# Attention with block turns: both scores of a slot ahead of the sums, sums in four visits, the norm a slot later, bias rows of the next heads first in the queue

## Chip, cores and metric

The kernel runs on one core of a Trainium2 chip. The metric is the device time of one launch in microseconds (us).

## What is computed

Attention with a position bias over 4 batches, 8 heads, 576 positions and a head size of 64, then two expert layers. Only the attention is touched here:

```
scores = q @ k.T / sqrt(D) + bias[head]        # 576 x 576 for each of 32 (batch, head)
attn   = exp(scores - max) / sum
out    = attn @ v
```

The bias depends on the head and on the two positions, not on the batch. A first stage of the kernel computes it for all heads and writes it to DRAM (`bias_ihj`).

## The kernel before, in words

**Pairs and passes.** Two heads of one batch form a pair; there are 16 pairs, and four pairs in a row (the four batches) share the bias rows of their two heads. Every engine runs `pair(p, ...)` for p = 0 to 15; the text calls one such call *pass p*. Passes 0, 1, 14 and 15 are written out, passes 2 to 13 are a loop of two passes a turn. Engines meet only through semaphores.

**Slots.** The 576 query rows of the two heads are cut into nine units of 128 rows: slots 0 to 3 hold one unit for each head, slot 4 (`MIX`) holds the last 64 rows of both. Work is one slot ahead: pass p makes slots 1, 2, 3 and MIX of pair p, then slot 0 of pair p+1. Under the same pass the weighted sums with V of pair p-1 are made.

**The steps of a unit**, with the lines of the profile:

- TensorE `scores` (L438): four matmuls for a unit, eight for MIX, into one of two PSUM buffers (h = 0, 1). A unit can start when the unit that used its buffer last has been read by VectorE.
- VectorE `add_bias` (L589): adds the bias, takes the row maximum, writes `a_sc` and `a_nmax`. The text calls it an *add*.
- ScalarE `exps` (L647): the exponential with its row sums, into `a_pr`.
- VectorE `turn` (L601): transposes 32 x 32 blocks of `a_pr` into `a_pt`.
- TensorE `values` (L547): the sums with V over 18 blocks of keys, 16 rows of the trace each. `VISITS` says in which slots of the pass which blocks are done. The first visit waits for V, for the turns of its pair, and for the norm of the pair before (`s_x`), whose PSUM banks it writes.
- ScalarE `keep_out` (L655, L661) copies the finished sums to `a_ot`, TensorE `turn_back` (L559) turns them into banks 4 and 5, and VectorE `normal` (L617, two products, the *norm*) multiplies them by the inverse row sums (L610, L611) into `a_xp`, which SyncE stores to `x_tokens`.

**GpSimd** splits q and k of a later pair in two parts (`split_k`, `split_q`, L367 to L387).

**SyncE's queue** issues all transfers in the order of the code: in pass p the q and k of pair p+2, in passes 3, 7 and 11 the five bias tiles of the next two heads (`load_bias`, L334, L331), the stores of pair p-1, and V of pair p+1 (`load_v`, L324). Each transfer of q, k or V is 288 KB, four for q and k of a pair and four for its V.

Of the kernel before, what the change touches and what calls it, by code (L numbers as in the profile page):

```python
# [275 lines left out]
def front_stages(sem, arena, psum, qt, kt, vt, ww, wg, biasd, xd, ident, rt, small):  # L276
# [7 lines left out]
    VISITS = {1: range(0, 6), 2: range(6, 12), 3: range(12, NK)}  # L284
# [161 lines left out]
    def sync(e):  # L446
# [18 lines left out]
        def pair(p, u, uses):  # L465
            if isinstance(p, int) and p == 0:
                load_v(e, 0, 0)
                load_v(e, 1, 1)
            if not (isinstance(p, int) and p >= NPAIR - 2):
                split_done(e, p)  # L470
                load_qk(e, p + 2, u)
            if not isinstance(p, int) and u == 1:
                with e.If(uses % 2 == 1):
                    for s in range(SLOTS):
                        e.wait_ge(s_b, sem.at(s_b, p * TPP + min(2 * s + 2, TPP)))
                        sem.apart(e, p)
                        load_bias(e, (p // B + 1) % (H // 2), s)
            if from_pair(p, 1):
                store_first(p - 1, 1 - u)
                if not (isinstance(p, int) and p == NPAIR - 1):  # L480
                    e.wait_ge(s_o, sem.at(s_o, p))
                    sem.apart(e, p)
                    load_v(e, p + 1, 1 - u)
                store_second(p - 1, 1 - u)

        each_pair(e, pair)
        store_first(NPAIR - 1, 1)
        store_second(NPAIR - 1, 1)
# [40 lines left out]
    def tensor(e):  # L529
# [34 lines left out]
        def pair(p, u, uses):  # L564
            for s in range(SLOTS):
# [3 lines left out]
                if s in VISITS and from_pair(p, 1):  # L569
                    values(p - 1, 1 - u, uses - 1 + u, VISITS[s])  # L570
                if exists(np_) and ns != MIX:
                    scores(e, np_, nu, nuses, ns, 1)
                if s == MIX and from_pair(p, 1):
                    turn_back(p - 1)
# [6 lines left out]
    def vector(e):  # L581
# [21 lines left out]

        def normal(p, u, uses, half):
# [3 lines left out]
            if half == 0:  # L608
                e.wait_ge(s_e, sem.at(s_e, p * TPP + TPP))
                e.reciprocal(rinv[:, u, 0:TPP], sums[:, u, :]).then_inc(s_r, 1)  # L610
                e.reciprocal(rinv[:, u, TPP:TPP + 1], sums[:, u, TPP - 1:TPP]).then_inc(s_r, 1)  # L611
# [9 lines left out]
        def pair(p, u, uses):  # L621
            for s in range(SLOTS):
# [3 lines left out]
                if exists(np_) and ns != MIX:  # L626
                    add_bias(np_, nu, nuses, ns, 1)
                turn(p, u, s)
                if s == MIX and from_pair(p, 1):
# [1186 lines left out]
```

## Time and profile before

| | |
|---|---|
| median of 3 runs | 1091.58 us (1091.49 to 1092.24) |
| profiled execution: its time, its span | 1093.94 us, 1092.1 us |
| busy over the span: TensorE, VectorE, ScalarE, GpSimd | 1006.4, 790.5, 413.6, 202.6 us |
| attention, from the first scores to the last norm | about 61 to 357 us of the span |
| mean granted TensorE clock | 0.966 |

Times in the rows are microseconds from the start of the span. PE is the matmul side of TensorE, PEld its weight loads, DVE is VectorE, ACT ScalarE, POOL GpSimd, and SPq SyncE's queue. The ends of matmuls are modelled by the profiler, their starts are not.

A row of busy time by stretch has the stretch, its length, then busy time and count of instructions of PE, PEld, DVE, ACT and POOL, the granted TensorE clock (1.00 is full), the busy share of the DMA engines, and GB/s.

A pass is counted here from the start of the add of its slot 1, head 0, to the same add of the next pass. These adds start at 77.51 us (pass 1), 123.89 (3), 230.77 (9), 246.11 (10), 313.54 (14) and 330.11 (15). The `turn_back` of pass 15 starts at 343.84 us.

### The profile page before, as it was taken

What the parts mean: (1) busy time and instruction counts of PE and PEld (TensorE: products, weight loads), DVE (VectorE), ACT (ScalarE), POOL (GpSimd) and SP (SyncE); (2) the same over time, 40 slices, a digit from 0 to 9 for tenths busy, and PEclk for the clock granted to TensorE, in tenths of its full rate; (3) what the DMA queues carried; (4) which work ended last, traced back from release to release, by engine and by line L of the source; (5) the groups of instructions that cost most, each with busy time, mean ns of one, the idle gap of its engine ahead of it and who ended that gap; (6) DMA issues with size and microseconds to landing.
All of it is one profiled execution on the core that took longest, in us unless ns stands there. A gap on an engine that the chain in (4) does not pass through costs nothing.

```text
span 1092.1 us, 28659 instructions
## 1 busy us (share of the span) xinstructions
PE 1006.4 (92%) x10409; PEld 913.6 (84%) x10410; DVE 790.5 (72%) x1268; ACT 413.6 (38%) x783; POOL 202.6 (19%) x195
## 2 busy tenths in 40 slices
PE   5876779798787999999999999999999999999997
PEld 2355667677677899999999999999999999999996
DVE  8985668688685845765656489878776777777765
ACT  7873445455453334644444244231121212112111
POOL 2025234525450231221212000001010100100101
PEclk9987989899898989999999999999999999999999
DMA  4886678878763581561512170002000100100000
GB/s 146 284 238 130 139 209 191 219 171 182 211 148 68 195 281 52 204 204 50 204 50 89 63 258 1 1 1 80 29 29 0 50 8 0 58 0 0 29 1 29
DMA packets 68078, 117.43 MB, mean 108 GB/s; under 512 B 28384, under 2 KB 39696, under 8 KB 65984
## 3 DMA queue, kind: packets, MB, share of 16 engines
q1 hardware_dynamic: 64000, 103.45, 33.9%
q0 software_dynamic: 4032, 13.37, 3.6%
q8 instruction: 28, 0.46, 0.2%
q14 instruction: 18, 0.15, 0.0%
HBM read 91.41 MB, written 25.40 MB: 107 GB/s over the span
## 4 chain that ended last, share of the span: by engine, by line
PE 65%; DVE 2%; issue 1%; ACT 1%; POOL 1%; DMA 0%; POOLq 0%; DVEq 0%; ACTq 0%
PE psum L1688 27%; PE psum L1696 13%; PE psum L1201 11%; PE psum L1210 10%; PE psum L1187 1%; PE psum L547 1%; DVE f_eg L1643 0%; PE psum L1249 0%; DMA e_xin<-x_tokens,e_col 0%; PE psum L559 0%; PE psum L831 0%; PE psum L849 0%; PE psum L438 0%; POOL e_xin L1153 0%; POOL e_col L1149 0%
## 5 line engine op out<-in xcount | busy, mean ns | idle before, releaser
L1643 DVE RECIPROCAL f_eg<-f_eg 128x384 f32<-128x384 f32 x72 | 183.3, 2545 | 0.0
L647 ACT ACTIVATE a_pr<-a_sc,a_nmax 128x576 f32<-128x576 f32 x144 | 111.3, 773 | 142.0 <-DVE a_nmax L589 96.1
L1611 ACT ACTIVATE f_eg<-psum 128x384 f32<-128x384 f32 x72 | 35.4, 492 | 312.0 <-PE psum L1688 312.0
L589 DVE CUSTOM_DVE_ANT_0 a_sc<-psum,a_bias 128x576 f32<-128x576 f32 x144 | 104.8, 743 | 65.3 <-PE psum L438 47.6
L1688 PE MATMUL psum<-f_x,f_ghi 128*128 (+1 forms) x576 | 147.5, 337 | 0.4 <-DVE f_x L1504 0.4
L1688 PE MATMUL psum<-f_x,f_vhi 128*128 (+1 forms) x576 | 146.1, 334 | 0.0
L438 PE MATMUL psum<-a_khi,a_qs 128*128 128x288 f32 x320 | 104.4, 345 | 34.7 <-DVE a_nmax L589 30.4
L438 PEld LDWEIGHTS psum<-a_khi,a_qs 128*128 128x128 f32 x320 | 65.1, 204 | 56.8 <-DVE a_nmax L589 40.8
L1688 PEld LDWEIGHTS psum<-f_x,f_ghi 128*128 128x128 f32 x576 | 105.8, 188 | 6.6 <-DVE f_x L1504 0.6
L547 PE MATMUL psum<-a_pt,a_v 32*64 32x128 f32 (+1 forms) x4608 | 102.0, 312 | 9.6 <-issue 8.8
L1580 POOL DMA_INDIRECT out<-f_ob,f_cols x18 | 18.1, 1007 | 464.9 <-ACT f_ob L1597 316.3
L547 PEld LDWEIGHTS psum<-a_pt,a_v 32*64 32x64 f32 x4608 | 86.3, 140 | 21.2 <-issue 21.2
L1688 PEld LDWEIGHTS psum<-f_x,f_vhi 128*128 128x128 f32 x576 | 104.0, 188 | 0.0
L601 DVE STREAM_TRANSPOSE a_pt<-a_pr 128x576 f32<-128x576 f32 x144 | 103.9, 756 | 0.0
L438 PE MATMUL psum<-a_klo,a_qs 128*128 128x288 f32 x320 | 94.1, 312 | 3.7 <-issue 3.7
L1688 PE MATMUL psum<-f_x,f_glo 128*128 (+1 forms) x288 | 97.1, 337 | 0.0
L1688 PE MATMUL psum<-f_x,f_vlo 128*128 (+1 forms) x288 | 96.2, 334 | 0.0
L1639 DVE TENSOR_SCALAR f_eg<-f_eg 128x384 f32<-128x384 f32 x72 | 26.4, 367 | 88.7 <-ACT f_eg L1611 88.7
L1210 PE MATMUL psum<-e_hhi,e_w2hi 128*128 128x288 f32 x288 | 87.4, 303 | 0.0
L1201 PE MATMUL psum<-e_xhi,e_w1hi 128*128 128x288 f32 x288 | 87.1, 303 | 0.0
L1696 PE MATMUL psum<-f_ohi,f_alo 128*128 128x512 f32 x216 | 85.4, 396 | 0.0
L1201 PE MATMUL psum<-e_xlo,e_w1hi 128*128 128x288 f32 x288 | 85.3, 296 | 0.0
(235 smaller groups left out, 2155.9 us busy)
## 6 DMA issues: line engine op xcount, KB each, us to landing
a_v<-v SPq DMA_DIRECT2D x64, 288.0 KB, 5.4
e_raw<-ew SPq DMA_DIRECT2D x16, 1024.0 KB, 5.2
bias_ihj<-b_res SPq DMA_DIRECT2D x36, 288.0 KB, 2.7
a_qraw<-q SPq DMA_DIRECT2D x32, 288.0 KB, 5.5
a_kraw<-k SPq DMA_DIRECT2D x32, 288.0 KB, 6.1
a_bias<-bias_ihj SPq DMA_DIRECT2D x16, 576.0 KB, 7.9
xn_t<-e_yn SPq DMA_DIRECT2D x8, 576.0 KB, 3.1
x_tokens<-a_xp SPq DMA_DIRECT2D x64, 64.0 KB, 2.0
```

What stands on the lines that cost most here:

```text
L438: mm = e.matmul(s_ps[:, h, half, 0:HALF], qs[:, u, c:c + P], k[:, u, a * S + half * HALF:a * S + (half + 1) * HALF], start=(i == 0), stop= ...
L547: mm = e.matmul(o_ps[64 * h:64 * h + 64, g, to:to + n], vv[rows, u, k, 64 * h:64 * h + 64], pt[rows, u, k, first:first + n], start=(k == 0 ...
L589: e.tensor_tensor_reduce(sc[:, h, :].rearrange("p (a s) -> p a s", a=2), s_ps[:, h, :, 0:HALF], bias[:, 2 * s + h, :].rearrange("p (c s) - ...
L601: t = e.transpose(pt[:, u, :, at:at + Q], pr[:, w, S * h:S * h + S].rearrange("p (k q) -> p k q", q=Q))
L647: mm = e.activation(pr[:, w, S * h:S * h + S], sc[:, h, :], ACT.Exp, bias=nmax[:, h:h + 1], scale=-1.0, accum_out=sums[:, u, 2 * s + h:2 * ...
L1201: mm = e.matmul(bank[:, 0:BT], w[:, k, :], x[:, u, k, :], start=(k == 0 and n == 0), stop=(k == KD - 1 and n == 2))
L1210: mm = e.matmul(banks.y[:, k, 0:BT], w[:, k * P:(k + 1) * P], h[:, f % 3, :], start=(f == 0 and n == 0), stop=(f == KF - 1 and n == 2))
L1611: e.activation(self.eg[:, k % 2, :], self.g_ps[k % 2][:, 0:CHUNK], ACT.Exp, scale=-1.0).then_inc(self.s_e, 1)
L1639: e.tensor_scalar(x, x, 1.0, None, ALU.add).then_inc(self.s_c, 1)
L1643: e.reciprocal(x, x).then_inc(self.s_c, 1)
L1688: mm = e.matmul(acc[:, 0:CHUNK], a, b, start=(q == 0 and i == 0), stop=(q == KD - 1 and i == 2))
L1696: mm = e.matmul(self.o_ps[t], x, y, start=(f == 0 and i == 0), stop=(f == KFF - 1 and i == 2))
```

## The change

The order of work inside a pass is changed on three engines. No operation is added to the arithmetic or taken from it.

- TensorE: both units of a slot come first, and the visit of `values` after them; it was between them. There are four visits of 3, 5, 5 and 5 blocks in slots 0 to 3; there were three of 6 blocks in slots 1 to 3.
- VectorE: the inverse row sums are taken by a function of their own, `inverse`, in slot 0 of the next pass. The norm of pair p-2 is made in slot 0 of pass p, behind the adds and ahead of the turns; it was at the end of pass p-1.
- SyncE: in pass p the bias tile of slot 0 comes first, then q and k, the stores of pair p-2, the other four bias tiles, and V. In pass 0, q and k of pair 2 go ahead of V.

```diff
-    VISITS = {1: range(0, 6), 2: range(6, 12), 3: range(12, NK)}
+    VISITS = (range(0, 3), range(3, 8), range(8, 13), range(13, NK))
...
         def pair(p, u, uses):
+            def next_bias(slots):
+                if not isinstance(p, int) and u == 1:
+                    with e.If(uses % 2 == 1):
+                        for s in slots:
+                            e.wait_ge(s_b, sem.at(s_b, p * TPP + min(2 * s + 2, TPP)))
+                            sem.apart(e, p)
+                            load_bias(e, (p // B + 1) % (H // 2), s)
+            next_bias((0,))
+            if not (isinstance(p, int) and p >= NPAIR - 2):
+                split_done(e, p)
+                load_qk(e, p + 2, u)
             if isinstance(p, int) and p == 0:
                 load_v(e, 0, 0)
                 load_v(e, 1, 1)
-            if not (isinstance(p, int) and p >= NPAIR - 2):
-                split_done(e, p)
-                load_qk(e, p + 2, u)
-            if not isinstance(p, int) and u == 1:
-                with e.If(uses % 2 == 1):
-                    for s in range(SLOTS):
-                        e.wait_ge(s_b, sem.at(s_b, p * TPP + min(2 * s + 2, TPP)))
-                        sem.apart(e, p)
-                        load_bias(e, (p // B + 1) % (H // 2), s)
-            if from_pair(p, 1):
-                store_first(p - 1, 1 - u)
-                if not (isinstance(p, int) and p == NPAIR - 1):
-                    e.wait_ge(s_o, sem.at(s_o, p))
-                    sem.apart(e, p)
-                    load_v(e, p + 1, 1 - u)
-                store_second(p - 1, 1 - u)
+            if from_pair(p, 2):
+                store_first(p - 2, u)
+                store_second(p - 2, u)
+            next_bias(range(1, SLOTS))
+            if from_pair(p, 1) and not (isinstance(p, int) and p == NPAIR - 1):
+                e.wait_ge(s_o, sem.at(s_o, p))
+                sem.apart(e, p)
+                load_v(e, p + 1, 1 - u)
...
                 if exists(np_):
                     scores(e, np_, nu, nuses, ns, 0)
-                if s in VISITS and from_pair(p, 1):
-                    values(p - 1, 1 - u, uses - 1 + u, VISITS[s])
                 if exists(np_) and ns != MIX:
                     scores(e, np_, nu, nuses, ns, 1)
+                if s != MIX and from_pair(p, 1):
+                    values(p - 1, 1 - u, uses - 1 + u, VISITS[s])
                 if s == MIX and from_pair(p, 1):
                     turn_back(p - 1)
...
+        def inverse(p, u):
+
+            e.wait_ge(s_e, sem.at(s_e, p * TPP + TPP))
+            e.reciprocal(rinv[:, u, 0:TPP], sums[:, u, :]).then_inc(s_r, 1)
+            e.reciprocal(rinv[:, u, TPP:TPP + 1], sums[:, u, TPP - 1:TPP]).then_inc(s_r, 1)
+
...
+                if s == 0 and from_pair(p, 2):
+                    for half in range(2):
+                        normal(p - 2, u, uses - 1, half)
                 turn(p, u, s)
-                if s == MIX and from_pair(p, 1):
-                    for half in range(2):
-                        normal(p - 1, 1 - u, uses - 1 + u, half)
+                if s == 0 and from_pair(p, 1):
+                    inverse(p - 1, 1 - u)
```

VectorE, slot 0 of the first pass of the loop, before: the two adds, with the turns right behind them.

```order
L589 ISA a_sc,a_nmax<-psum,a_bias 128x576
L589 ISA a_nmax 128x1
L585 REGISTER_ALU
L586 REGISTER_ALU
L589 ISA a_sc,a_nmax<-psum,a_bias 128x576
L589 ISA a_nmax 128x1
L597 REGISTER_ALU
L601 STREAM_TRANSPOSE a_pt<-a_pr 128x18x32 x2
```

The same place of the change (L593 is the add now, L605 the turn, L624 the norm).

```order
L593 ISA a_sc,a_nmax<-psum,a_bias 128x576
L593 ISA a_nmax 128x1
L619 ISA
L621 REGISTER_ALU
L622 ISA
L623 REGISTER_ALU
L624 TENSOR_TENSOR a_xp<-psum,a_rinv 128x288
L622 ISA
L624 TENSOR_TENSOR a_xp<-psum,a_rinv 128x432
L601 REGISTER_ALU
L605 STREAM_TRANSPOSE a_pt<-a_pr 128x18x32 x2
```

The two products of the norm stand between the adds and the turns now.

TensorE, the first visit of `values` in that pass, before: it follows the scores of slot 2, head 0 (L534 to L538 are its waits).

```order
L433 REGISTER_ALU
L438 MATMUL psum<-a_khi,a_qs 128x288
L438 MATMUL psum<-a_klo,a_qs 128x288
L438 MATMUL psum<-a_khi,a_qs 128x288
L438 MATMUL psum<-a_klo,a_qs 128x288
L534 ISA
L535 ISA
L538 ISA
L547 MATMUL psum<-a_pt,a_v 64x160
```

The change: it follows the scores of slot 1, head 1 (L538 to L542 are the same waits, L551 is `values`).

```order
L433 REGISTER_ALU
L438 MATMUL psum<-a_khi,a_qs 128x288
L438 MATMUL psum<-a_klo,a_qs 128x288
L438 MATMUL psum<-a_khi,a_qs 128x288
L438 MATMUL psum<-a_klo,a_qs 128x288
L538 ISA
L539 ISA
L542 ISA
L551 MATMUL psum<-a_pt,a_v 64x160
```

The first visit, with its wait for the norm, has moved one slot forward, and the norm one slot back.

SyncE, the start of the second pass of the loop, in the change: the branch with the bias tile of slot 0 stands ahead of q and k.

```order
L468 ISA
L468 COMPARE_AND_BRANCH
L470 ISA
L334 ISA
L334 DMA a_bias<-bias_ihj 128x1152
L468 UNCONDITIONAL_BRANCH
L317 ISA
L317 DMA a_qraw<-q 64x1152
```

Before, that tile came behind the q and k of the same pass, and those behind the stores and the V of the pass ahead of it.

## Rows read from the trace of the kernel before

**Rows 1.** Busy time by stretch: pass 9, passes 1-2, 3-13, and 14.

```profile
230.77:246.11 15.34, 13.46 (x338) 11.58 (x338) 13.56 (x33) 8.79 (x22) 6.75 (x4) 1.00 0.78 173
77.51:123.89 46.38, 33.52 (x680) 28.84 (x678) 27.41 (x63) 16.94 (x43) 21.55 (x13) 0.81 0.58 127
123.89:313.54 189.65, 157.08 (x3718) 134.53 (x3718) 148.74 (x342) 93.71 (x232) 80.58 (x52) 0.93 0.82 196
313.54:330.11 16.57, 13.46 (x338) 11.53 (x338) 13.45 (x32) 8.36 (x22) 11.07 (x23) 1.00 0.42 91
```

**Rows 2.** Timeline of VectorE, pass 9 and the norm ahead of it: start, duration.

```profile
229.88 0.97 DVE L617 TENSOR_TENSOR a_xp<-psum,a_rinv 128x288 f32<-128x288 f32 x2 [0.31 <-PE psum L559]
230.77 0.74 DVE L589 CUSTOM_DVE_ANT_0 a_sc<-psum,a_bias 128x576 f32<-128x576 f32 x1
...
233.48 0.72 DVE L589 CUSTOM_DVE_ANT_0 a_sc<-psum,a_bias 128x576 f32<-128x576 f32 x1
...
235.16 0.76 DVE L589 CUSTOM_DVE_ANT_0 a_sc<-psum,a_bias 128x576 f32<-128x576 f32 x1 [0.94 <-PE psum L438]
...
240.30 0.72 DVE L589 CUSTOM_DVE_ANT_0 a_sc<-psum,a_bias 128x576 f32<-128x576 f32 x1
```

**Rows 3.** Timeline of TensorE's matmuls in pass 9.

```profile
231.58 0.40 PE L438 MATMUL psum<-a_khi,a_qs 128*128 128x288 f32 x1 [0.95 <-DVE a_nmax L589]
...
232.30 1.91 PE L547 MATMUL psum<-a_pt,a_v 32*64 32x160 f32 x96
...
234.14 0.40 PE L438 MATMUL psum<-a_khi,a_qs 128*128 128x288 f32 x1
...
237.98 0.40 PE L438 MATMUL psum<-a_khi,a_qs 128*128 128x288 f32 x1
...
239.25 1.91 PE L547 MATMUL psum<-a_pt,a_v 32*64 32x160 f32 x96
...
243.16 1.49 PE L559 MATMUL psum<-a_xw,a_ot 128*128 x10 [0.67 <-ACT a_ot L661]
...
244.39 0.39 PE L438 MATMUL psum<-a_khi,a_qs 128*128 128x288 f32 x1
```

**Rows 4.** Timeline of ScalarE at the end of pass 9.

```profile
241.14 0.78 ACT L647 ACTIVATE a_pr<-a_sc,a_nmax 128x576 f32<-128x576 f32 x1 [1.21 <-DVE a_nmax L589]
...
242.03 0.60 ACT L655 ACTIVATE a_ot<-psum 128x512 f32<-128x512 f32 x1
```

**Rows 5.** VectorE's waits for bias tiles, 60 to 360 us: total, times, longest.

```profile
DVE a_sc L589 <- DMA a_bias<-bias_ihj: 15.7, 3, 6.2
```

**Rows 6.** Bias tiles: issue in pass 7 on SyncE's timeline; KB and landing on the page.

```profile
202.45 2.43 SPq L334 DMA_DIRECT2D a_bias<-bias_ihj  x4
...
a_bias<-bias_ihj SPq DMA_DIRECT2D x16, 576.0 KB, 7.9
```

**Rows 7.** Timelines at the end of pass 15: the norm, and the sums that wait for it.

```profile
345.98 0.61 DVE L617 TENSOR_TENSOR a_xp<-psum,a_rinv 128x432 f32<-128x432 f32 x1 [0.83 <-PE psum L559]
...
346.73 7.42 PE L547 MATMUL psum<-a_pt,a_v 32*64 32x160 f32 x288 [0.79 <-DVE a_xp L617]
```

**Rows 8.** Longer gaps of TensorE's matmuls, on its timeline.

```profile
112.06 2.66 PE L547 MATMUL psum<-a_pt,a_v 32*64 32x128 f32 x77 [3.50 <-issue]
...
321.68 0.29 PE L547 MATMUL psum<-a_pt,a_v 32*64 32x160 f32 x1 [1.63 <-issue]
...
343.84 2.10 PE L559 MATMUL psum<-a_xw,a_ot 128*128 128x144 f32 x10 [1.83 <-ACT a_ot L661]
```

**Rows 9.** Busy time just behind the last and the first of these gaps.

```profile
345.00:347.50 2.50, 1.71 (x32) 1.39 (x35) 0.90 (x4) 0.00 (x0) 0.35 (x1) 0.50 0.22 52
112.50:115.50 3.00, 3.00 (x71) 2.56 (x54) 0.00 (x0) 0.00 (x0) 0.00 (x0) 0.50 0.83 178
```

**Rows 10.** The start: V of pairs 0 and 1 on SyncE's queue; VectorE in pass 1.

```profile
69.18 4.07 SPq L324 DMA_DIRECT2D a_v<-v  x8
...
98.69 0.76 DVE L589 CUSTOM_DVE_ANT_0 a_sc<-psum,a_bias 128x576 f32<-128x576 f32 x1 [6.74 <-PE psum L438]
```

More of the change, by code:

```diff
@@ L468, in pair @@
                 load_v(e, 1, 1)
-            if not (isinstance(p, int) and p >= NPAIR - 2):
-                split_done(e, p)
-                load_qk(e, p + 2, u)
-            if not isinstance(p, int) and u == 1:
-                with e.If(uses % 2 == 1):
-                    for s in range(SLOTS):
-                        e.wait_ge(s_b, sem.at(s_b, p * TPP + min(2 * s + 2, TPP)))
-                        sem.apart(e, p)
-                        load_bias(e, (p // B + 1) % (H // 2), s)
-            if from_pair(p, 1):
-                store_first(p - 1, 1 - u)
-                if not (isinstance(p, int) and p == NPAIR - 1):
-                    e.wait_ge(s_o, sem.at(s_o, p))
-                    sem.apart(e, p)
-                    load_v(e, p + 1, 1 - u)
-                store_second(p - 1, 1 - u)
+            if from_pair(p, 2):
[6 more added lines that the diff above has]
+                load_v(e, p + 1, 1 - u)
         each_pair(e, pair)
-        store_first(NPAIR - 1, 1)
-        store_second(NPAIR - 1, 1)
+        for p in (NPAIR - 2, NPAIR - 1):
+            store_first(p, p % 2)
+            store_second(p, p % 2)
         for u in range(2):
@@ L608, in normal @@
             if half == 0:
-                e.wait_ge(s_e, sem.at(s_e, p * TPP + TPP))
-                e.reciprocal(rinv[:, u, 0:TPP], sums[:, u, :]).then_inc(s_r, 1)
-                e.reciprocal(rinv[:, u, TPP:TPP + 1], sums[:, u, TPP - 1:TPP]).then_inc(s_r, 1)
                 e.wait_ge(s_r, sem.at(s_r, p * 2 + 2))
@@ L635, in vector @@
         each_pair(e, pair)
+        for half in range(2):
+            normal(NPAIR - 2, 0, NPAIR // 2 - 1, half)
+        inverse(NPAIR - 1, 1)
         for half in range(2):
```

## Prediction, made blind

> **What bounds the attention now.** I read the page first: TensorE is the busiest engine over the span, but that is the expert layers' doing. Busy time by stretch then shows pass 9, a pass with nothing unusual in it [rows 1]: 15.34 us, VectorE busy 13.56, TensorE 13.46, clock 1.00. Neither engine fills it; the two take turns in waiting. VectorE's timeline shows where. Between the adds of slot 2 it waits 0.94 us for scores [rows 2], because TensorE does a visit of sums, six blocks, between the two units of the slot (scores at 231.58, sums at 232.30, next scores at 234.14) [rows 3]. Smaller waits, like the 0.31 us ahead of the norm, make the rest of the 1.8 us. In three passes VectorE waits for a bias tile as well, 15.7 us in all [rows 5]: in pass 7 the tiles are issued at 202.45 and take about 7.9 us to land, behind q and k [rows 6].
>
> **What the change takes away.** (a) The bias waits. The slot 0 tile may be replaced once slot 0 of its pair is added, at the end of the pass before, and SyncE now stands there with nothing ahead of it: it is issued some 13 us before its use, against 7.9 us to land. The other four follow the stores, 6 to 10 us into the pass; the first is used about 17 us into it. I cost the waits at nothing afterwards. If q and k, which are on their way then, delayed them by 3 us more, there would still be none. (b) With both units ahead of the sums, the 0.94 us goes. (c) The inverse row sums no longer stand in the norm's way.
>
> **What it adds.** The norm of pair p-2 now comes behind the two adds of slot 1, and the first visit of sums waits for it. I follow one pass at full clock; t = 0 is the add of slot 1, head 0.
>
> - The second add ends at 1.36 (two adds and two turns take 2.71, 230.77 to 233.48, or 0.68 each) [rows 2]. The norm's two products take 0.89 together (229.88 to 230.77) [rows 2]; the second starts 0.36 after the first, at 1.72. From the start of the second product to the sums that wait for it: 0.75 (345.98 to 346.73) [rows 7]. Sums start at 2.47.
> - Six blocks take 1.61 (1.91 less the 0.30 of the last matmul) and 0.23 more until the next scores, 1.84 in all [rows 3]. So three blocks take 1.03, five 1.57. Eight score matmuls take 1.27 up to the sums behind them (237.98 to 239.25), four take 0.72.
> - Scores of slot 2 start at 3.50, of slot 3 at 3.50 + 1.27 + 1.57 = 6.34, of MIX at 9.18. VectorE needs less: an add starts 1.02 after the start of its unit's scores (234.14 to 235.16) [rows 2, 3] and the slot's two adds and two turns take 2.7, against 2.84 of TensorE. TensorE is the chain from here.
> - The add of MIX: 9.18 + 1.02 + 0.55 for four more matmuls = 10.75. Its exponential starts 0.84 later (240.30 to 241.14), the copy of the sums 0.89 after that, `turn_back` 1.13 after that, the next pass's scores 1.23 later, their add 1.02 later [rows 2 to 4]: 15.86.
>
> So at full clock a pass takes 15.86 us and not 15.34. What TensorE waited for in small pieces it now waits for in one: its eight scores are done at about t = 0.3 and the sums start at 2.47. **A gap of about 2.2 us** opens in every pass.
>
> **What the gap does to the clock.** In the steady passes the gap ahead of the scores was 0.95 and the clock stayed at 1.00 [rows 1, 3]. A gap of 1.83 us ahead of `turn_back` was followed by 0.50, 1.2 GHz [rows 8, 9]; a gap of 3.50 as well; a gap of 1.63 us was not (pass 14 shows 1.00) [rows 1, 8]. The new gap lies beyond the one that was followed by half clock, so I take one fall in each pass. It hits the part where TensorE is the chain. Its price: 77 of the matmuls of the sums took 2.66 us at half clock, where 77/96 of 1.91 = 1.53 would do: 1.74 times as long. The shortest slow stretch in the trace runs at least from 112.06 to 115.5, 3.44 us [rows 8, 9]; it loses 3.44 x (1 - 1/1.74) = 1.46. A pass is then 15.86 + 1.46 = 17.3 us. Bounds: no fall, 15.86; a slow stretch of twice the length, 18.8.
>
> The Trainium skill ("TensorE: Matmul & The Clock Gate", HAM oscillation) speaks against this: the idle gaps of which it warns are all longer than 2.2 us. By it a pass would stay at 15.86. The row with 1.83 us does not agree with it, and I go by the row.
>
> **The sum**, against the profiled execution (its own time is 1093.94 us, span 1092.1; the median of the runs is 1091.58, and I apply the difference to the median):
>
> - Passes 3 to 13: 11 x 17.3 = 190.3, before 189.65 [rows 1]: +0.7. The 15.7 us of bias waits and the slow stretches that followed them pay for nearly all of the longer passes.
> - Pass 14: 17.3 plus the 1.6 us gap that TensorE has there on no other engine's account (at 321.68) [rows 8] = 18.9, before 16.57: +2.3.
> - Pass 15 up to its `turn_back`: 13.61 in my chain, plus what this pass lost before against pass 9, (343.84 - 330.11) - (243.16 - 230.77) = 1.34: 14.95, before 13.73: +1.2.
> - Passes 1 and 2, 46.38 before. The 6.74 us in which VectorE waited for scores whose q was not split yet [rows 10] go, as q and k of pair 2 are no longer behind 2.3 MB of V. In their place V of pair 0 comes behind them: its issue starts at about 71.7 instead of 69.18, and 1.15 MB at some 196 GB/s [rows 1] is 5.9 us, so it lands at about 82, where the first sums could start at 79. That gap of 3 us costs itself and a slow stretch, 4.5. The gap at 112.06 stays. The longer pass 2 adds 0.5, the other small terms 0.4. Together -1.3, with bounds -5 and +3.
>
> +0.7 + 2.3 + 1.2 - 1.3 = +2.9: 1091.6 + 2.9 = **1094.5 us**. Behind pass 15 nothing moves: the last sums, norm and stores follow in the same order.
>
> **The rivals.**
>
> - *The clock stays full* (17 in 100). For it: the gap of 1.63 us did no harm, and mine is a sum of eight durations. Against it: 1.83 us did. Passes 3 to 13 take 11 x 15.86 = 174.5, -15.2; pass 14 17.5, +0.9; pass 15 +1.2; passes 1 and 2 -3: 1075.5. It decides at a gap between 1.63 and 1.83.
> - *It falls, but not in every pass, or the chain is shorter than mine* (11 in 100): half the falls give 12 x 0.73 = 8.8 less, 1085.7.
> - *Slow stretches twice as long*, since the next gap may find the clock still low (8 in 100): 12 x 1.46 = 17.5 more, 1112. In the stretch behind 343.84 work went on at half clock, which speaks for it; that TensorE works without a pause for 13 us of each pass speaks against.
> - *The bias wait only moves to slot 1* (2 in 100): 3 x 4 us more, 1106.5.
>
> That leaves 62 in 100 for the forecast, whose own range is 1089 to 1101: the lower bound of passes 1 and 2 gives 3.7 less, their upper bound and 0.2 us a pass more give 6.7 more.
>
> **Numbers.** A measurement of this kernel tells about 0.2%, 2.2 us, from no change. Slower than 1093.8: both slow rivals and 40 of the forecast's 62, 50. Faster than 1089.4: the first two rivals and the edge of the forecast's range, 28. Between: 22. The range goes from 1076, which takes in the half falls and part of the full clock, to 1102.
>
> **What the trace will show.** Right: no wait for a bias tile; the add of slot 1 waiting about 0.7 us for scores and the adds of one slot back to back; sums of the first visit that wait for the norm, 2.2 us idle; a granted clock of 0.85 to 0.92 over the loop with one slow stretch a pass; passes of 17 to 17.6 us. Wrong: 1.00 over the loop with passes near 15.9 is the first rival, passes near 15.2 mean that the chain through the norm is not there. What would upset the forecast most is the clock: all but 3 us of the distance between 1075 and 1094 hangs on it.

## The result

| | before | changed |
|---|---|---|
| median (lowest to highest) | 1091.91 us (1091.49 to 1092.85, 4 runs) | 1101.07 us (1099.54 to 1108.15, 4 runs) |
| profiled execution: time, span | 1093.94, 1092.1 us | 1099.54, 1097.7 us |
| mean granted TensorE clock | 0.966 | 0.963 |

The change makes the kernel slower: the ratio is 1.0095, with a 95% interval of 1.0051 to 1.0139. That is 9.2 us where 2.9 were forecast. The profiled execution of the changed kernel is the quickest of its four and the one of the kernel before lies 2 us above the median there, so the two spans differ by less, 5.6 us.

Busy time by stretch on TensorE, for the changed kernel: the stretch, its length, busy time and count, granted clock, DMA share, GB/s. The stretches are pass 9, passes 1 and 2, pass 3, passes 4 to 13, and pass 14; the ones of before stand in [rows 1], which has passes 3 to 13 as one.

```profile
234.81:252.56 17.75, 15.26 (x341) 0.90 0.72 153
77.61:127.18 49.57, 36.19 (x679) 0.79 0.61 132
127.18:148.48 21.30, 14.53 (x341) 1.00 0.94 253
148.48:320.63 172.15, 145.51 (x3378) 0.92 0.81 185
320.63:337.37 16.74, 14.75 (x340) 0.90 0.40 87
```

Pass 9 takes 17.75 us and had 15.34. Passes 4 to 13 take 17.2 us on average, at 0.92 of the clock. VectorE's timeline in pass 9 shows the new order, the old one stands in [rows 2]:

```profile
234.81 0.76 DVE L593 CUSTOM_DVE_ANT_0 a_sc<-psum,a_bias 128x576 f32<-128x576 f32 x1 [0.48 <-ACT a_pr L659]
...
235.49 0.75 DVE L593 CUSTOM_DVE_ANT_0 a_sc<-psum,a_bias 128x576 f32<-128x576 f32 x1
...
236.17 0.97 DVE L624 TENSOR_TENSOR a_xp<-psum,a_rinv 128x288 f32<-128x288 f32 x2
237.06 1.43 DVE L605 STREAM_TRANSPOSE a_pt<-a_pr 128x576 f32<-128x576 f32 x2
...
239.60 0.76 DVE L593 CUSTOM_DVE_ANT_0 a_sc<-psum,a_bias 128x576 f32<-128x576 f32 x1 [0.99 <-PE psum L438]
```

The norm stands behind the adds of slot 1. TensorE's matmuls in the same place, and its waits of 60 to 360 us (in total, times, longest):

```profile
237.29 1.08 PE L551 MATMUL psum<-a_pt,a_v 32*64 32x160 f32 x48 [2.16 <-DVE a_xp L624]
238.29 0.40 PE L438 MATMUL psum<-a_khi,a_qs 128*128 128x288 f32 x1
238.53 0.36 PE L438 MATMUL psum<-a_klo,a_qs 128*128 128x288 f32 x1
238.69 0.44 PE L438 MATMUL psum<-a_khi,a_qs 128*128 128x288 f32 x1
...
PE psum L551 <- DVE a_xp L624: 33.4, 15, 2.8
PE psum L551 <- issue: 11.0, 5, 3.0
PE psum L551 <- DMA a_v<-v: 4.9, 1, 4.9
```

The first visit of sums starts at 237.29, 2.48 us behind the add of slot 1 (234.81), after 2.16 us without a matmul. About 1.2 us later the score matmuls go from 0.29 to 0.44 us each: the clock has gone to its lower level, 1.2 GHz. Fourteen first visits wait like this; the fifteenth wait in the row is the last one, of 0.79 us, which the kernel before had too. No wait for a bias tile is left.

TensorE's other gaps lie in passes 1 to 3:

```profile
83.24 1.91 PE L551 MATMUL psum<-a_pt,a_v 32*64 32x160 f32 x48 [4.89 <-DMA a_v<-v]
...
95.25 0.81 PE L551 MATMUL psum<-a_pt,a_v 32*64 32x128 f32 x9 [3.00 <-issue]
...
137.89 1.34 PE L551 MATMUL psum<-a_pt,a_v 32*64 32x128 f32 x61 [2.40 <-issue]
...
143.90 0.77 PE L551 MATMUL psum<-a_pt,a_v 32*64 32x160 f32 x22 [2.18 <-issue]
```

In pass 1 the V of pair 0 comes 4.89 us late. Pass 3 took 21.30 us (21.57 before): two gaps in it have no releaser ("issue"). The text calls such a gap a *stop*.

### The profile page after: what moved, and what is told of

Same layout as the page of the kernel before. It is cut to its first block, busy times and chain, and to the rows that moved or that the text cites. A ratio compares the mean times of both kernels' runs of the same rounds, so it can differ in the third digit from the quotient of the medians.

```text
span 1097.7 us, 28662 instructions
## 1 busy us (share of the span) xinstructions
PE 1014.5 (92%) x10409; PEld 921.0 (84%) x10410; DVE 793.3 (72%) x1268; ACT 411.2 (37%) x783; POOL 204.8 (19%) x195
## 4 chain that ended last, share of the span: by engine, by line
PE 84%; issue 4%; DVE 3%; DMA 3%; ACT 3%; DVEq 1%; SPq 0%; ACTq 0%; POOL 0%; POOLq 0%
PE psum L1700 27%; PE psum L1708 13%; PE psum L1213 10%; PE psum L1222 10%; PE psum L551 10%; PE psum L438 8%; DMA bias_ihj<-b_res 2%; PE psum L563 2%; PE psum L1199 1%; DVE a_xp L624 1%; DMA a_v<-v 1%; PE psum L843 1%; ACT b_hid L234 1%; ACT a_ot L667 1%; ACT b_res L244 1%
## 5 line engine op out<-in xcount | busy, mean ns | idle before, releaser
L593 DVE CUSTOM_DVE_ANT_0 a_sc<-psum,a_bias 128x576 f32<-128x576 f32 x144 | 105.0, 755 | 75.2 <-PE psum L438 72.4
L551 PE MATMUL psum<-a_pt,a_v 32*64 32x128 f32 (+1 forms) x4608 | 108.8, 316 | 49.3 <-DVE a_xp L624 33.4
L551 PEld LDWEIGHTS psum<-a_pt,a_v 32*64 32x64 f32 x4608 | 87.7, 143 | 62.5 <-issue 57.1
L438 PE MATMUL psum<-a_khi,a_qs 128*128 128x288 f32 x320 | 107.7, 354 | 4.3 <-DVE a_nmax L593 4.2
L1592 POOL DMA_INDIRECT out<-f_ob,f_cols x18 | 18.1, 1006 | 465.0 <-ACT f_ob L1609 316.3
L605 DVE STREAM_TRANSPOSE a_pt<-a_pr 128x576 f32<-128x576 f32 x144 | 103.9, 756 | 0.0
L438 PE MATMUL psum<-a_klo,a_qs 128*128 128x288 f32 x320 | 98.0, 324 | 0.0
L438 PEld LDWEIGHTS psum<-a_khi,a_qs 128*128 128x128 f32 x320 | 68.8, 215 | 22.9 <-issue 17.6
L1708 PE MATMUL psum<-f_olo,f_ahi 128*128 128x512 f32 x216 | 85.3, 395 | 0.0
```

The lines of the kernel that those rows point to most:

```text
L438: mm = e.matmul(s_ps[:, h, half, 0:HALF], qs[:, u, c:c + P], k[:, u, a * S + half * HALF:a * S + (half + 1) * HALF], start=(i == 0), stop= ...
L551: mm = e.matmul(o_ps[64 * h:64 * h + 64, g, to:to + n], vv[rows, u, k, 64 * h:64 * h + 64], pt[rows, u, k, first:first + n], start=(k == 0 ...
L593: e.tensor_tensor_reduce(sc[:, h, :].rearrange("p (a s) -> p a s", a=2), s_ps[:, h, :, 0:HALF], bias[:, 2 * s + h, :].rearrange("p (c s) - ...
L605: t = e.transpose(pt[:, u, :, at:at + Q], pr[:, w, S * h:S * h + S].rearrange("p (k q) -> p k q", q=Q))
L1708: mm = e.matmul(self.o_ps[t], x, y, start=(f == 0 and i == 0), stop=(f == KFF - 1 and i == 2))
```

## The experiments

The theory after the result: (1) in each pass the first visit of sums waits for the norm of its own slot, and behind that gap the clock falls; (2) bias rows first in the queue are a gain of their own; (3) the start loses time to V. The rivals were that a later norm or four visits cost by themselves, that only the 2 us of waiting count and not the clock, or that the bias rows are worth little.

All twelve runs in one table: the lengths are read from the starts of VectorE's adds in the profiled execution of each; "gap" is TensorE's longest usual wait in a pass of the loop (two values where passes differ), "clock" the granted clock from 160 to 300 us. Runs were made beside the kernel before, which had medians of 1092.33 to 1092.89 us there; differences of two rows are of medians unless a trace is named.

| kernel | us | ratio (interval) | passes 1-3 | mean of 4-13 | gap | clock |
|---|---|---|---|---|---|---|
| before | 1091.91 | | 67.9 | 16.81 | 0.95, 1.2 | 0.93 |
| changed | 1101.07 | 1.0095 (1.0051-1.0139) | 70.9 | 17.22 | 2.2, 2.7 | 0.90 |
| norm at the end | 1059.95 | 0.9706 (0.9669-0.9743) | 69.4 | 13.96 | 0.3 | 1.00 |
| 12 fillers | 1080.76 | 0.9891 (0.9853-0.9930) | 66.5 | 15.98 | 0.9 | 1.00 |
| V first | 1094.49 | 1.0021 (0.9996-1.0046) | 66.2 | 16.94 | 2.2, 2.6 | 0.93 |
| SyncE's order only | 1072.93 | 0.9821 (0.9784-0.9859) | 69.7 | 15.35 | 0.95, 1.2 | 1.00 |
| sums in slots 1 to 3 | 1063.27 | 0.9730 (0.9696-0.9764) | 63.4 | 14.62 | 0.9 | 1.00 |
| order of scores only | 1101.12 | 1.0075 (1.0053-1.0098) | 68.3 | 17.33 | 1.6, 1.9 | 0.89 |
| 6 fillers | 1082.96 | 0.9905 (0.9876-0.9934) | 65.9 | 16.13 | 1.4, 1.7 | 0.99 |
| norm at the end, V first | 1055.38 | 0.9659 (0.9624-0.9694) | 63.3 | 13.96 | 0.3 | 1.00 |
| no reload of bias rows | 1096.74 | 1.0032 (1.0018-1.0046) | 70.5 | 16.92 | 2.2, 2.4 | 0.93 |
| norm at the end, sums 1 to 3 | 1061.58 | 0.9721 (0.9692-0.9751) | 65.0 | 14.49 | 1.1 | 1.00 |
| norm and reciprocals later, queue | 1079.65 | 0.9869 (0.9846-0.9891) | 68.7 | 15.83 | 0.9 | 0.99 |
| the same with reciprocals at the end | 1082.57 | 0.9904 (0.9878-0.9930) | 69.2 | 16.53 | 1.6, 1.9 | 0.91 |

("The same" in the last line is the version with norm at the end and sums in slots 1 to 3. "No reload" leaves a part of the computation out: all heads use the bias rows of the first two.)

### 1. The norm back at the end of its pass

```diff
-                if s == 0 and from_pair(p, 2):
-                    for half in range(2):
-                        normal(p - 2, u, uses - 1, half)
                 turn(p, u, s)
                 if s == 0 and from_pair(p, 1):
                     inverse(p - 1, 1 - u)
+                if s == MIX and from_pair(p, 1):
+                    for half in range(2):
+                        normal(p - 1, 1 - u, uses - 1 + u, half)
...
         each_pair(e, pair)
-        for half in range(2):
-            normal(NPAIR - 2, 0, NPAIR // 2 - 1, half)
```

> The change with the norm put back to the end of the pass (the inverse row sums stay in slot 0 of the next pass). Theory: the wait of the first visit of sums for the norm makes the 2.2 us gap, and the gap makes the clock fall. Then both go: passes 4 to 13 of about 13.7 us instead of 17.2, clock 1.00 in them, 12 passes x 3.5 = 42 us less than the change: 1055 to 1065 us. Rival: the order of TensorE's work (both scores ahead of the sums, four visits) is what makes the passes long. Then the passes stay above 15.2 and the time above 1080.

Measured: 1059.95 us. One line of TensorE's timeline in the place of the wait:

```profile
244.36 1.07 PE L551 MATMUL psum<-a_pt,a_v 32*64 32x160 f32 x48 [0.21 <-DVE a_xp L624]
```

The wait of 2.16 us is 0.21. The first visit now stands beside the adds of slot 1 and fills TensorE there. One moved call is worth 41 us and turns the change from a loss into a gain of 32 us over the kernel before.

### 2 and 3. Is it the waiting or the clock? Work put into the gap

```diff
+                if s == 0 and from_pair(p, 2):
+                    for i in range(12):
+                        e.matmul(o_ps[:, 2 + i % 2, 0:HALF], qs[:, u, 0:P], khi[:, u, 0:HALF],
+                                 start=True, stop=True)
                 if s != MIX and from_pair(p, 1):
                     values(p - 1, 1 - u, uses - 1 + u, VISITS[s])
```

The filler does nothing useful; the sums behind it overwrite its banks.

> The change with 12 extra score-sized matmuls on TensorE between the second scores of slot 1 and the first visit of sums, written to a bank that nothing reads until it is overwritten: work that leads to nothing, about 1.6 us of it inside the gap. Theory: the gap costs twice, by the wait (0.7 us a pass) and by the clock (1.3 us on average). The filler takes the second away only: clock 1.00 in passes 4 to 13, passes of 15.9 to 16.1, 1085 to 1090 us. Rival: the clock is harmless and the wait is all: 1099 to 1103, passes of 17.2.

Measured: 1080.76 us, better than expected. The norm is as late as before and the pass is still 15.98 us, which is the chain of the forecast at full clock (15.86). The clock is 1.00 in the loop. Compared with the changed kernel, the passes 4 to 13 shorten by 172.2 - 159.8 = 12.4 us though nothing was taken out: that is what the clock costs there. The rest of the 20 us is in passes 1 to 3 (4.4), pass 14 (16.74 to 15.22), and in the spread of the runs. The part in passes 1 to 3 is not the clock's alone: pass 2 has none of its stops here and is 5.5 us shorter.

With 6 in place of 12:

> The changed kernel with six added matmuls of 128x288 ahead of the first visit of the sums, in place of the twelve of the run with fillers; nothing reads what they write. Six take about 1.8 us at full clock, so some 0.4 us of the wait for the norm stays in each pass, and the filler costs no pass any time. Theory (what costs most is the clock that falls behind a long gap): most falls are gone, passes of 15.9 to 16.4 us, 1078 to 1087 us. Rival (the twelve helped in another way, by holding back the sums or the DMAs): a gain of half of theirs or less, 1090 us or more.

Measured: 1082.96 us. Six fillers take 0.8 us (the shorter gap goes from 2.16 to 1.36), not the 1.8 of the expectation. Gaps of 1.35 to 1.71 us are left in each pass, and in one of the passes 4 to 13 the clock falls:

```profile
176.25 1.07 PE L551 MATMUL psum<-a_pt,a_v 32*64 32x160 f32 x48 [1.71 <-DVE a_xp L628]
...
240.36 1.08 PE L551 MATMUL psum<-a_pt,a_v 32*64 32x160 f32 x48 [1.71 <-DVE a_xp L628]
```

Busy time of TensorE just behind these two gaps, in the same trace:

```profile
176.20:179.20 3.00, 2.95 (x97) 1.00 1.03 215
240.30:243.30 3.00, 2.94 (x64) 0.75 1.02 217
```

The same gap was followed by full clock once and by a fall once. Half the filler gives nine tenths of the gain (18.1 of 20.3 us; 10.9 of 12.4 in passes 4 to 13), so the time is not proportional to the gap; the number of falls decides.

### 4. The V loads of the start first

```diff
         def pair(p, u, uses):
             ...
+            if isinstance(p, int) and p == 0:
+                load_v(e, 0, 0)
+                load_v(e, 1, 1)
             next_bias((0,))
             if not (isinstance(p, int) and p >= NPAIR - 2):
                 split_done(e, p)
                 load_qk(e, p + 2, u)
-            if isinstance(p, int) and p == 0:
-                load_v(e, 0, 0)
-                load_v(e, 1, 1)
```

> The change with V of pairs 0 and 1 ahead of q and k of pair 2 in the queue of pass 0, as before. Theory: the late V idles TensorE for 4.9 us in pass 1 and leaves it at half clock behind it; with V first this goes and the wait for the split of q of pair 2 comes back, so pass 1 moves by -4 to 0 us from its 27.9 and the rest stays: 1096 to 1101 us. Rival: the start is what lies between the forecast and the result: 1094 or less.

Measured: 1094.49 us, between the two expectations: 6.6 us less than the changed kernel. The profiled execution is the lowest of its ten (1089.32 us) and lies 10.2 us below the one of the changed kernel: 4.7 us in passes 1 to 3 (70.9 to 66.2), 2.8 in passes 4 to 13, whose falls of the clock are not the same ones in each trace (six in place of seven, none of them long), and 1.5 in pass 14. The wait for V in pass 1 is gone, but pass 1 shortens by 1.3 us only (27.86 to 26.52); pass 2, which has no stop here, by 4.3.

### 5. SyncE's order alone, in the kernel before

The `pair` of `sync` and the stores behind it as in the diff of the change, all else as before.

> The kernel before with the change's order of SyncE's queue alone. Theory: the three bias waits (15.7 us) and the slow stretches behind them (5 us) go, the start moves by -4 to +2: 1068 to 1076 us. Rival: what the queue brings is lost in the start and in gaps of TensorE's own in pass 3 (two of 2.2 to 2.4 us in the change): 1080 or more.

Measured: 1072.93 us. The order is worth more than the 15.7 us of waiting for bias rows, since the half clock behind those waits goes with them: 1.00 in place of 0.93 in the loop. Yet pass 3, which had one of the three bias waits, is no shorter: 22.33 us (21.57 before). TensorE's and VectorE's timelines of this kernel in pass 3:

```profile
132.57 1.88 PE L551 MATMUL psum<-a_pt,a_v 32*64 32x128 f32 x41 [3.72 <-issue]
...
135.93 0.76 DVE L593 CUSTOM_DVE_ANT_0 a_sc<-psum,a_bias 128x576 f32<-128x576 f32 x1 [5.84 <-PE psum L438]
```

TensorE stops in the middle of a visit, with nothing to wait for, and VectorE waits 5.84 us for the scores behind it. For comparison the kernel before in the same pass: TensorE's busy time from 123.89 to 145.46 us, VectorE's wait for a bias tile, and TensorE's two stops.

```profile
123.89:145.46 21.57, 14.97 (x338) 0.95 0.93 246
...
DVE a_sc L589 <- DMA a_bias<-bias_ihj: 4.7, 1, 4.7
...
130.89 1.05 PE L547 MATMUL psum<-a_pt,a_v 32*64 32x128 f32 x41 [1.07 <-issue]
...
136.52 0.77 PE L547 MATMUL psum<-a_pt,a_v 32*64 32x160 f32 x22 [1.27 <-issue]
```

The wait of 4.7 us went, and stops of 2.3 us became one of 3.7 with a longer wait of VectorE behind it.

### 6. The sums moved away from the norm instead

```diff
-    VISITS = (range(0, 3), range(3, 8), range(8, 13), range(13, NK))
+    VISITS = {1: range(0, 6), 2: range(6, 12), 3: range(12, NK)}
...
-                if s != MIX and from_pair(p, 1):
+                if s in VISITS and from_pair(p, 1):
                     values(p - 1, 1 - u, uses - 1 + u, VISITS[s])
```

> The changed kernel with the sums of the pair before moved out of slot 0: visits of six key blocks in slots 1, 2 and 3, as before the change, while both scores stay ahead and the norm stays one slot later. Theory (the first visit in slot 0 waits for the norm of the same slot, and TensorE's clock falls behind that wait): by slot 1 the norm has long been written, so the 33.4 us of waits of the sums for a_xp are gone, the granted clock of the loop is 1.0, and the passes 4 to 13 take 14.3 to 14.9 us in place of 17.2; time 1065 to 1078 us. Rival 1 (the norm one slot later costs by itself, by holding VectorE ahead of the turn): passes of 16 us or more, 1085 to 1095 us. Rival 2 (four visits fill TensorE better than three): the gap goes but the passes stay near 15.9, 1080 to 1087 us.

Measured: 1063.27 us. The mirror of experiment 1 has nearly the same effect: of the later norm and the sums in slot 0 neither loses the time, only both in one slot. The start gains as well (63.4 us in passes 1 to 3); the wait for V of pair 0 is 2.76 us in place of 4.89.

### 7. The order of the scores alone, in the kernel before

```diff
-                if s in VISITS and from_pair(p, 1):
-                    values(p - 1, 1 - u, uses - 1 + u, VISITS[s])
                 if exists(np_) and ns != MIX:
                     scores(e, np_, nu, nuses, ns, 1)
+                if s in VISITS and from_pair(p, 1):
+                    values(p - 1, 1 - u, uses - 1 + u, VISITS[s])
```

> The kernel before with one edit: both scores of a slot stand ahead of the sums on TensorE; visits of six blocks in slots 1 to 3, norm at the end of the pass, SyncE's order as before. Theory (of the four parts of the change the order of scores and sums is a gain of its own, some 0.9 us in a pass by the bare sums of the rows; the bias waits of 15.7 us stay): 1077 to 1084 us. Rival 1 (it gives nothing while the bias rows come late): 1090 to 1093 us. Rival 2 (it gives all that the version with the norm at the end of the pass gave over the kernel before, less the bias waits): 1072 to 1077 us.

Measured: 1101.12 us, slower than before, and no expectation had that. TensorE's timeline in pass 6, and ScalarE's:

```profile
177.87 0.43 PE L438 MATMUL psum<-a_khi,a_qs 128*128 128x288 f32 x1 [1.94 <-DVE a_nmax L589]
178.10 0.43 PE L438 MATMUL psum<-a_klo,a_qs 128*128 128x288 f32 x1
...
190.12 1.49 PE L559 MATMUL psum<-a_xw,a_ot 128*128 x10
...
192.31 0.78 ACT L647 ACTIVATE a_pr<-a_sc,a_nmax 128x576 f32<-128x576 f32 x1 [2.38 <-DVE a_rinv L611]
```

The first scores of slot 2 can only start when the first add of slot 1 has been made, and that add stands behind the reciprocals and the norm. TensorE has no sums to do in slot 0, waits 1.94 us, and its clock falls there (0.43 us a matmul). All this was so in the order of before too, where the same wait was 0.95 us in pass 9; but there TensorE waited another 0.67 us for ScalarE's copy ahead of `turn_back` [rows 3]. Now ScalarE's copy is done in time, `turn_back` at 190.12 waits for nothing, and the whole wait stands in one place: 1.62 us in pass 9, which is 0.95 + 0.67. At full clock the order changes nothing (pass 5 takes 15.32 us here and 15.35 before). What it costs is the falls: in nine of the passes 4 to 13 the clock is low for a time, where it was in five before, all five at or behind the late bias tiles.

### 8. The two edits of 1 and 4 together

> Norm back at the end of its pass and the V loads of pairs 0 and 1 ahead of q and k of pair 2. The two edits alone gave 1059.95 and 1094.49 us. Theory (independent: the V wait of 5.6 us of TensorE in pass 1 and the half clock behind it go): 1051 to 1056 us. Rival (TensorE's own stops in passes 1 to 3, or the late q and k of pair 2, take the wait's place): 1058 to 1061 us.

Measured: 1055.38 us, the fastest version of this case, 3.4% less than before. Passes 1 to 3 take 63.3 us where the norm at the end alone has 69.4. In the loop VectorE waits 4.0 us for scores from 160 to 280 us and for little else; it is the bound there now. Without the late V (experiment 1 against this one) pass 1 shortens by 2.4 us and pass 2 by 3.7.

### 9. Are TensorE's stops in pass 3 due to the bias rows?

```diff
-            next_bias((0,))
...
-            next_bias(range(1, SLOTS))
...
-            e.wait_ge(s_bias[s], sem.at(s_bias[s], (p // B + 1) * (32 if s == MIX else 16)))
+            e.wait_ge(s_bias[s], sem.at(s_bias[s], 32 if s == MIX else 16))
```

> The changed kernel without the loads of the bias rows of later heads (all heads use the rows of the first two, so that this part of the computation is left out; SyncE issues 18 transfers fewer, in passes 3, 7 and 11). It asks why pass 3 took 21.3 us where 17.3 were forecast. Theory: TensorE's own stops of 2.40 and 2.18 us in that pass are loads of instructions that stand in the DMA engines behind the bias rows; with these gone the stops shrink to 1 us or less and pass 3 takes 17 to 19 us, passes 7 and 11 stay at 17.8, time 1096 to 1099 us. Rival 1 (the stops are the time that a load of instructions takes by itself): pass 3 stays at 20.5 us or more, time 1100 to 1103 us. Rival 2 (the bias rows slow q, k and V in all three passes): passes 3, 7 and 11 each shorten by 1 us or more, 1093 to 1096 us.

Measured: 1096.74 us. TensorE's timeline in pass 3:

```profile
139.35 1.34 PE L549 MATMUL psum<-a_pt,a_v 32*64 32x128 f32 x61 [1.36 <-issue]
```

Pass 3 fell to 19.37 us, with one stop of 1.36 in place of 2.40 and 2.18. But pass 2 rose to 23.76 (21.71), and passes 1 to 3 together stay at 70.5. The stops of pass 3 add up to 1.4 us here, and to 2.3 to 4.8 in every other trace of the case, so the bias rows may lengthen the stops beside them; they are not what makes the start long as a whole, and the theory of this run holds for one pass only. The gain of 4 us lies in the loop, where the clock falls in seven of the passes 4 to 13 as in the changed kernel, but never for as long as in its pass 8 (18.78 us).

### 10 to 12. What made the order of the scores slow

These three runs ask why the order of the scores was a loss in experiment 7. Norm at the end (experiment 1) and sums in slots 1 to 3 (experiment 6) in one kernel:

> The changed kernel with the norm back at the end of its pass and with the sums in slots 1 to 3, so that of the change the order of the scores and SyncE's order remain. Each of the two edits alone removed the wait: 1059.95 and 1063.27 us. Theory, from the run with the order alone (1101.12 us): then TensorE has nothing in slot 0 but scores while VectorE does the norm and the turns of the last slots, waits 1.6 to 1.9 us for the adds ahead of the second scores of slot 1, and its clock falls there; passes of 16.3 to 16.9 us in most of the loop, time 1082 to 1092 us. Rival (the run with the order alone was slow only by the late bias rows, and the two edits add up): passes under 14.7 us, time 1050 to 1063 us.

Measured: 1061.58 us, and the theory fell. TensorE's timeline:

```profile
201.37 0.40 PE L438 MATMUL psum<-a_khi,a_qs 128*128 128x288 f32 x1 [1.11 <-DVE a_nmax L593]
```

The gap is there, but it is 1.11 us and not 1.9, and the clock stays full. (The text of the expectation calls the waiting scores the second ones of slot 1; the rows show that they are the first ones of slot 2.) What this kernel has beside the order of the scores is SyncE's order, with the bias rows in time, and the reciprocals in slot 0. So the last run moved the reciprocals back:

```diff
                 turn(p, u, s)
-                if s == 0 and from_pair(p, 1):
-                    inverse(p - 1, 1 - u)
                 if s == MIX and from_pair(p, 1):
+                    inverse(p - 1, 1 - u)
                     for half in range(2):
                         normal(p - 1, 1 - u, uses - 1 + u, half)
```

> The version with norm at the end and sums in slots 1 to 3 (1061.58 us), with the two reciprocals moved from slot 0 to just ahead of the norm, where they stood before the change. It asks why the order of the scores alone gave 1101.12 us although that order is part of three versions near 1060 us. Theory: with the reciprocals ahead of the norm in the last slot, exp of the next pair's first scores waits for them (2.38 us in the trace of the order alone) and the norm ends some 0.8 us later, TensorE's wait ahead of the second scores of slot 1 grows from 1.1 to 1.6 to 1.9 us, and its clock falls there in most passes; 15.3 to 16.9 us a pass, time 1076 to 1090 us. Rival (the late bias rows alone made that run slow): passes of 14.5 to 14.8 us, 1061 to 1066 us.

Measured: 1082.57 us, 21 us more for two instructions of 0.17 and 0.10 us moved by one slot. TensorE's waits at three places of its timeline:

```profile
181.40 0.40 PE L438 MATMUL psum<-a_khi,a_qs 128*128 128x288 f32 x1 [1.90 <-DVE a_nmax L593]
...
197.97 0.40 PE L438 MATMUL psum<-a_khi,a_qs 128*128 128x288 f32 x1 [1.62 <-DVE a_nmax L593]
...
231.51 0.40 PE L438 MATMUL psum<-a_khi,a_qs 128*128 128x288 f32 x1 [1.61 <-DVE a_nmax L593]
```

and its busy time behind each:

```profile
181.40:184.40 3.00, 3.00 (x60) 0.70 0.96 203
198.00:201.00 3.00, 3.00 (x68) 0.78 0.91 252
231.50:234.50 3.00, 2.99 (x102) 1.00 0.96 201
```

The norm has to wait for the reciprocals' result, all of VectorE's work behind it comes later, and the gap grows from 1.1 to 1.6 and 1.9 us. The clock falls behind most of them, in nine of the ten passes. The one pass without a fall takes 15.28 us (14.50 in the version before this one), so of the 20.4 us in passes 4 to 13 about 8 are the longer chain and the other 12 to 13 the clock. That is the loss of experiment 7; SyncE's order would account for the 18.6 us between the two, as it does between the kernel before and SyncE's order alone (19.4).

The change without its order of scores and sums, that is the later norm and reciprocals and SyncE's order:

> The changed kernel with the scores and the sums in the order of before (the second scores of a slot behind a visit, visits of six blocks in slots 1 to 3), so that of the change the later norm and SyncE's order remain; SyncE's order alone gave 1072.93 us. Theory (the later norm costs only where sums stand behind it in its slot; here the first visit is a slot away): passes of 14.9 to 15.4 us as with SyncE's order alone or a little less, no fall of the clock in the loop, 1064 to 1074 us. Rival (the norm in slot 0 delays the turn of slot 0 and by it exp and the sums): passes of 16 us or more, 1080 us or more.

Measured: 1079.65 us, between the two expectations. TensorE's first visit in pass 9, and its busy time in pass 10:

```profile
226.37 1.89 PE L551 MATMUL psum<-a_pt,a_v 32*64 32x160 f32 x96 [0.85 <-DVE a_xp L624]
```

```profile
242.50:245.50 3.00, 3.00 (x97) 0.51 1.05 221
```

The theory had the first visit a slot away from the norm and the wait at nothing. The rows show that it is not far enough: the visit stands ahead of the second scores of slot 2, and waits 0.85 us for the norm in each pass. A pass takes 15.83 us where SyncE's order alone has 15.35. Where both scores come first (experiment 6) the same wait is 0.17 us. No wait of TensorE in its loop is longer than 0.86 us, and yet the clock falls once, in pass 10, which takes 17.18 us. So the later norm and reciprocals are a loss of 6.7 us in this order of the scores, and of 1.7 us in the new one (1063.27 against 1061.58).

## Why the forecast was wrong

**The mechanism was right.** The bias waits are gone; the first visit waits 2.2 us for the norm in each pass (2.16 at 237.29); it starts 2.48 us after the add of slot 1 (2.47 worked out from [rows 2, 7]). The passes in which the clock stayed full took 16.03 to 16.07 us, and 15.69 for pass 13 (15.86 worked out). The passes 4 to 13 take 172.15 us, where ten times 17.3 were forecast.

**The clock.** One fall in a pass at 1.46 us was taken from the shortest slow stretch [rows 8, 9]. The passes of the loop with a fall take 17.2 to 17.8 us (one 18.78), those without 16.05, so a fall costs 1.2 to 1.7 us; three of the passes 4 to 13 have none. All falls together cost 12.4 us where 14.6 were forecast, and a pass at full clock is 15.98 us (12 fillers) and not 15.86. The errors cancel, which is luck. The forecast said that nearly all of the distance to 1075 hangs on the clock; the fillers bear it out in the main: with the same late norm and full clock the kernel takes 1080.76 us.

Two terms of the sum failed, both ahead of the steady passes.

**The first step that failed is pass 3.** The sum took it for a pass of the loop, 17.3 us, once its bias wait was gone. It took 21.30: +4.0 us on the term "passes 3 to 13". The wait of 4.7 us did go. But TensorE's own stops in this pass, 1.07 and 1.27 us before, were 2.40 and 2.18 us, and VectorE waited for the scores behind them. The forecast had the stops of passes 2 and 14 in its rows and left those of pass 3 out. Experiment 5 shows it without any other part of the change: the wait goes, a longer stop takes its place, the pass is as long as ever. In the other two places the bias waits were worth what was forecast: passes 7, 8, 11 and 12 are 14.5 us shorter in experiment 5 than before.

What are these stops? In every trace of the case TensorE has them in passes 1 to 3, none in passes 4 to 13, and in some again in passes 14 and 15 ([rows 8], 321.68). These are the places where it runs code for the first time: passes written out, and the first turn of the loop. They make a pass long: where pass 2 had none (V first, 6 and 12 fillers) it took 16.3 to 17.4 us, in all other traces 18.9 to 23.8. The DMA queues of the changed kernel show transfers of instructions from 77 to 165 us (packets, MB, share); from 165 to 300 us there is no such line:

```profile
q8 instruction: 8, 0.13, 0.6%
q14 instruction: 5, 0.04, 0.2%
```

One of these transfers of 16 KB goes with each stop. In the changed kernel those of q8 begin at 92.49, 113.00, 135.25 and 141.58 us, and the stops at 92.25, 113.29, 135.49 and 141.72. In all fourteen traces each of the 50 stops of over 0.9 us ends 1.3 to 1.8 us behind the end of a transfer on q8, and the longest, 5.35 us with the norm at the end, is the one whose transfer begins latest, 2.7 us into the stop. This speaks strongly for instructions that come late. No run took the stops away by themselves, so it is argued from the times and not shown by an experiment. Not every such transfer has a stop beside it, and why some come too late, and why pass 2 had no stop in three kernels, stays open. The bias rows are not seen to slow the transfers themselves: the one ahead of the stop of pass 3 took 1.17 us in experiment 9, those of the changed kernel 1.33 and 1.06.

**The second is passes 1 and 2, the larger of the two.** Forecast -1.3 us, with bounds of -5 and +3; measured 49.57 - 46.38 = +3.2, so the term was 4.5 us off. The wait for V was 4.89 us and not 3 (sums at 83.24, not 82), and behind it TensorE ran at half clock. Behind the other stops of these passes (95.25, 3.00 us) the clock was low too. The forecast had -1.3 because it credited the 6.74 us of the q split [rows 10] in full; but pass 1 grew from 25.65 to 27.86 us: V and TensorE's stop took its place. What V's place costs by itself is known in part only: experiment 4 gives 6.6 us on the median; in its trace pass 1, where the wait was, is shorter by 1.3 us, and pass 2, which has no stop there, by 4.3.

**Pass 14 and 15.** Forecast +2.3 and +1.2, measured +0.17 and, up to `turn_back`, 352.09 - 337.37 = 14.72 against 13.73, +1.0. TensorE's own stop at 321.68 has no counterpart in pass 14 of the changed kernel. From that `turn_back` to the end of the attention the changed kernel saves 1.4 us: the gap ahead of `turn_back`, behind which the clock had fallen, is 1.14 us in place of 1.83, and the sums that follow ran at full clock. Another 1.3 us goes in the expert layers, which the change does not touch.

The sum in the profiled executions: +0.1 at the start, +3.2 (passes 1, 2), -0.3 (pass 3), +4.1 (4 to 13), +0.2, +1.0, then -2.7 up to the end: +5.6 of span. Against the forecast the two failed terms gave +8.5, and what came out lower than forecast (passes 4 to 13, 14, 15 and the end) took 5.9 of it back. The medians differ by 9.2 us, 3.6 more than the profiled executions: the one of before lay 2.0 us above its median, the one of the changed kernel 1.5 below. That part has no row.

**The rule of the skill.** The Trainium skill ("TensorE: Matmul & The Clock Gate", HAM oscillation) would have kept the clock full at such gaps. The runs here say otherwise: 2.17 and 2.16 us were followed by half clock, so were some of 1.6 to 1.9 us, and once it fell with no wait over 0.9 us.

**What each part is worth.** SyncE's order: -19.4 us. Both scores ahead of the sums: +8.5 us alone, but -16 us where reciprocals, norm and sums leave it room (1063.27 against 1079.65). Reciprocals in slot 0: -21 us with it. Norm later: +7 us with the old order of the scores, +2 with the new one. Norm later and the first visit in the same slot: +41 us against the norm at the end, and this is what makes the change a loss.

## What to carry to other kernels

When two engines hand work to each other in turn, price a moved step by what the other engine can do meanwhile: the norm cost TensorE nothing where a visit of sums lay beside it, and 41 us where that visit waited for it. A long piece of waiting is worse than the same waiting in small pieces, as the clock tends to fall behind it: 1.62 us in one piece had falls in most passes, 0.95 and 0.67 us had none. Keep independent work for the gap, or break it up. And before crediting a wait that goes, look at what else the same pass was late by: passes that run code for the first time have stops of their own, and one of these can take the place of the wait.

## What the runs showed of the hardware

- The length of a gap alone does not tell whether TensorE's clock falls behind it. In the changed kernel 2.70 us at 151.15 were followed by full clock and 2.17 us at 167.02 by half; TensorE's matmuls there, and its busy time behind each:

```profile
151.15 1.07 PE L551 MATMUL psum<-a_pt,a_v 32*64 32x160 f32 x48 [2.70 <-DVE a_xp L624]
...
167.02 1.91 PE L551 MATMUL psum<-a_pt,a_v 32*64 32x160 f32 x48 [2.17 <-DVE a_xp L624]
```

```profile
151.10:154.10 3.00, 2.95 (x97) 1.00 1.02 214
167.00:170.00 3.00, 2.98 (x53) 0.50 0.96 203
```

- The clock can fall with no wait of over 0.9 us near. In the kernel with norm and reciprocals later and SyncE's order, two waits of 0.85 and 0.86 us up to 242.25 were followed by half clock in pass 10 (0.51 from 242.50 to 245.50), and much the same waits in the other nine of the passes 4 to 13 by full clock.
- Two reciprocals of 0.17 and 0.10 us, moved by one slot, changed the time by 21 us: they made a pass 0.8 us longer at full clock, and turned a gap of 1.1 us into one of 1.6 to 1.9 in each pass, behind which the clock fell in nine of ten.
- In code that runs for the first time TensorE stops for up to 5.4 us at a time, and each stop of over 0.9 us, in every trace of the case, ends 1.3 to 1.8 us behind a transfer of 16 KB of instructions on queue q8; in passes 4 to 13 there is no such stop of over 0.3 us, and from 3 us into pass 4 up to pass 14 no such transfer.
